# Two constant masks of an attention stage held in float32 in place of float16

## The reference

```
k_n = k / (norm(k) + 1e-6)
y[t] = q[t] @ state
v_old = k_n[t] @ state
state = state + beta[t] * outer(k_n[t], v[t] - v_old)
```

## Time and profile before

| | us |
|---|---|
| median of 3 runs | 1160.63 (1160.08 to 1163.29) |
| the profiled execution | 1159.56 |
| its span, first to last instruction | 1157.8 |
| TensorE matmul busy | 1044.8 (90%) |
| VectorE busy | 640.2 (55%) |
| ScalarE busy | 496.4 (43%) |
| GpSimd busy | 403.1 (35%) |
| mean granted TensorE clock | 0.931 |

### The profile page before, as it was taken

One profiled execution on the slowest core, in us unless ns is written; L12 is line 12 of the kernel. 1 busy time (PEld: TensorE's weight loads), 2 busy tenths in 40 slices (PEclk: granted clock), 3 DMA queues, 4 the chain that ended last, 5 costly groups with the idle time before them and its releaser, 6 DMA issues. The chain is left out here.

```text
span 1157.8 us, 28648 instructions
## 1 busy us (share of the span) xinstructions
PE 1044.8 (90%) x10998; PEld 898.0 (78%) x10998; DVE 640.2 (55%) x1051; ACT 496.4 (43%) x1007; POOL 403.1 (35%) x333
## 2 busy tenths in 40 slices
PE   3899898998989985999999999999994699999997
PEld 2788787888878874788787878878782588988886
DVE  5676576776777753645344343534435555445555
ACT  3564455655555643444233333423331434333433
POOL 5656446456546431005023050501302523212223
PEclk9798789988889987999999999999997799999999
DMA  9223333223330004401010010100000813444423
GB/s 149 61 52 65 69 75 63 45 58 71 68 76 16 16 16 134 154 1 55 0 55 0 0 54 0 54 0 27 0 0 27 273 64 123 140 163 163 149 93 112
DMA packets 135378, 79.38 MB, mean 69 GB/s; under 512 B 78414, under 2 KB 126038, under 8 KB 135286
## 3 DMA queue, kind: packets, MB, share of 16 engines
q1 hardware_dynamic: 132886, 73.27, 23.4%
q10 hardware_dynamic: 2400, 4.72, 1.1%
HBM read 63.03 MB, written 14.94 MB: 67 GB/s over the span
## 5 line engine op out<-in xcount | busy, mean ns | idle before, releaser
L1170 DVE SCALAR_TENSOR_TENSOR m_act_r<-m_act_r,m_sb_col 128x512 f32<-128x512 f32 x96 | 84.0, 875 | 144.2 <-ACT m_act_r L1097 144.2
L1488 POOL TENSOR_TENSOR e_w_lo<-e_w_raw,e_w_hi 128x384 fp32r<-128x384 f32 x64 | 72.6, 1144 | 177.2 <-ACT e_w_hi L1510 177.2
L1097 ACT ACTIVATE m_act_r<-m_hid 128x512 f32<-128x512 f32 x96 | 57.0, 594 | 142.1 <-PE m_hid L1215 140.2
L1173 DVE SCALAR_TENSOR_TENSOR m_g_lo<-m_act_r,m_sb_col,m_g_hi 128x512 fp32r<-128x512 f32 x96 | 75.5, 786 | 76.0 <-ACT m_g_hi L1100 76.0
L1215 PE MATMUL m_hid<-m_x_hi,m_w_hi 128*128 128x512 f32 x288 | 113.1, 393 | 4.3 <-DVE m_x_lo L1158 4.3
L1100 ACT ACTIVATE m_g_hi<-m_act_r,m_sb_col 128x512 fp32r<-128x512 f32 x96 | 69.5, 724 | 102.6 <-DVE m_act_r L1170 102.6
L1215 PE MATMUL m_out<-m_g_hi,m_w_hi 128*128 128x512 f32 x288 | 112.9, 392 | 0.5 <-DVE m_g_lo L1173 0.3
L1045 POOL TENSOR_TENSOR m_sq<-m_x_f 128x512 f32<-128x512 f32 x15 | 15.2, 1041 | 282.0 <-ACT m_x_f L1107 282.0
L1215 PE MATMUL m_hid<-m_x_lo,m_w_hi 128*128 128x512 f32 x288 | 112.9, 392 | 0.0
L1215 PE MATMUL m_hid<-m_x_hi,m_w_lo 128*128 128x512 f32 x288 | 112.8, 392 | 0.0
L1215 PE MATMUL m_out<-m_g_hi,m_w_lo 128*128 128x512 f32 x288 | 112.2, 390 | 0.0
(11 more groups left out here) (225 smaller groups left out, 2674.4 us busy)
## 6 DMA issues: line engine op xcount, KB each, us to landing
e_w_raw<-in_moe_w_dram SPq DMA_DIRECT2D x64, 384.0 KB, 7.1
a_b_rows<-in_beta_dram SPq DMA_DIRECT2D x48, 128.0 KB, 3.6
e_x_raw<-x2T_scratch SPq DMA_DIRECT2D x8, 768.0 KB, 4.7
out_dram<-e_acc SPq DMA_DIRECT2D x7, 768.0 KB, 3.5
a_k_raw<-in_k_dram SPq DMA_DIRECT2D x24, 192.0 KB, 3.8
a_q_raw<-in_q_dram SPq DMA_DIRECT2D x48, 96.0 KB, 3.0
a_v_raw<-in_v_dram SPq DMA_DIRECT2D x24, 192.0 KB, 3.6
xT_scratch<-a_y_T SPq DMA_DIRECT2D x48, 96.0 KB, 2.0
```

What stands on the lines that cost most here:

```text
L1097: nc.scalar.activation(act_r[:, f % RING, :], hid[f % RING][:, :], ACT.Relu).then_inc(s["relu_ready"], 1)
L1170: nc.vector.scalar_tensor_tensor(out=r, in0=r, scalar=sb_col[:, 0:1], in1=r, op0=ALU.mult, op1=ALU.mult).then_inc(s["sq_ready"], 1)
L1173: nc.vector.scalar_tensor_tensor(out=g_lo[:, f % RING, :], in0=r, scalar=sb_col[:, 1:2], in1=f32(g_hi[:, f % RING, :]), op0=ALU.add, op1=A ...
L1488: nc.gpsimd.tensor_tensor(w1_lo[:, :, c], w1_raw[:, :, c], f32(w1_hi[:, :, c]), ALU.subtract).then_inc(s["w1_lo_ready"], 1)
```

## The change

Two masks are held in float32. `minus_small` replaces `minus_small_h` and is made in float32; `off_blocks` reads `upper_off`, which is there in float32 already, in place of its float16 copy. The copy `upper_off_h` is still made. The outputs stay float16, and the values of the masks are 0, 1 and -1 in both types.

```diff
-        minus_small_h = sb("a_minus_small_h", [C, C], F16)
+        minus_small = sb("a_minus_small", [C, C], F32)
...
-            nc.vector.tensor_scalar(minus_small_h[:, :], small_blk[:, :], -1.0, None, ALU.mult).then_inc(s["made_v"], 1)
+            nc.vector.tensor_scalar(minus_small[:, :], small_blk[:, :], -1.0, None, ALU.mult).then_inc(s["made_v"], 1)
...
-                    nc.vector.tensor_tensor(l_small[:, gs(g), :], l_hi[:, gs(g), :], blk(minus_small_h), ALU.mult
+                    nc.vector.tensor_tensor(l_small[:, gs(g), :], l_hi[:, gs(g), :], blk(minus_small), ALU.mult
                                             ).then_inc(sg["l_small"][i], 1)
...
-                    nc.vector.tensor_tensor(l_offT[:, gs(g), :], l_hi[:, gs(g), :], blk(upper_off_h), ALU.mult
+                    nc.vector.tensor_tensor(l_offT[:, gs(g), :], l_hi[:, gs(g), :], blk(upper_off), ALU.mult
                                             ).then_inc(sg["l_offT"][i], 1)
```

## The result

The changed kernel takes 1173.72 us (median of 4 runs, 1172.81 to 1174.53), the kernel before beside it 1161.86. The ratio is 1.0095, with a 95% interval from 1.0074 to 1.0116: 11 us, or about 1%, slower. The forecast was 14.6 us or 1.3% slower, 1175.2. The two profiled executions lie 14.6 us apart (1159.56 and 1174.12), but that this is the forecast's own number is chance: the profiled execution of the kernel before lies 2.3 us under its median, that of the changed kernel 0.4 above.

A forecast was written before the change was run, and what follows sets the result against it. TensorE was taken to set the pace in the attention stage, standing still 62 of 442 us, partly for VectorE. Terms 8.4 + 4.2 + 2.0 = 14.6 us gave 1174.2 profiled, 1175.2 as median; range 1160 to 1192.

The forecast's parts named there:

- The bare price: Each of 48 VectorE mask products takes 0.54 us more, 1.22 alone, 1.09 behind GpSimd; 26 us of VectorE time.
- rival 4: The mixed float16 and float32 product is no slower, or all is hidden: 1160.6 us; chance 0.12.
- The first race: Second `l_small` against GpSimd's `l_lo` in A phases: VectorE wins, `l_small` ends almost 1 us earlier, `l_lo` takes 3.17.
- A phases: Seven of the attention stage's eleven phases, those not at the rolled loop's edge: 7 x 1.2 = 8.4 us.
- the prologue: From 25.38 us on, both `off_blocks` end later (30.1 for 28.6, 32.5 for 30.5): 2.0 us.
- B phases: Four phases at the rolled loop's edge: GpSimd keeps the lead, residual 1.06 late, 4 x 1.06 = 4.2 us.
- The second race: Second `off_blocks` against the other `l_lo` in A phases: GpSimd wins by 0.16 us, third `small_out` 1.2 us late.
- rival 1: VectorE wins the second race too, an A phase costs only 0.25: 1168.6 us; chance 0.20.
- TensorE's waits: Attention stage: wait for `l_small` gone, for `residual` above 2 us, a new one for `small_out` near 1 us.
- The clock: TensorE's granted clock in the attention stage, mean 0.87, left as it is in the sum.
- rival 2: More half clock in the attention stage: 10 us on top if half-clock time grows by a third, 1185 us; chance 0.18.
- rival 3: Faster: `l_small` wait and clock fall go in A phases, 1149.7 us with all seven; chance 0.08.

The follow-up runs named there:

- repeated run: The changed kernel, unaltered, run again beside its variants: 1172.39 us, 1.0099 of the kernel before.
- second pair: Kernel before and changed kernel, GpSimd's `vb` first, `l_lo` of group 1 waiting for `off_blocks` of group 1: 1126.94 us (float16), 1135.24 us (float32).
- first pair: Kernel before and changed kernel, GpSimd's `vb` first, `l_lo` of group 1 waiting for `off_blocks` of group 0: 1128.62 us (float16), 1137.70 us (float32).

## Why the prediction was right

**The bare price** was taken at 1.22 us alone and 1.09 behind GpSimd, from the experts' float32 rows. Measured 1.216 and 1.09. One float32 input is enough to lose the float16 pace; rival 4 falls. The Trainium skill's Vector Engine (DVE) Microarchitecture Reference, section 5.1, asks for two bytes in every source and the destination before a product of two tensors runs at two elements a cycle, and the trace agrees (1.216 us for the mix, 0.683 for float16 alone).

**The first race** was to go to VectorE in A phases, by a tie seen once in the prologue. It did in all seven, with `l_small` at 1.23, `l_lo` at 3.08 to 3.17 (forecast 3.17) and `vb` at 2.45 (forecast 2.46). The B phases went as written, `l_small` waiting and `off_blocks` ending 1.08 behind `vb`.

**The second race** was to go to GpSimd by 0.16 us in all seven. It went to GpSimd in five; in the two others VectorE was 0.01 us ahead, as at 170.79 against 170.80:

```profile
170.79 1.21 DVE L534 TENSOR_TENSOR a_t_small_x<-a_l_hi,a_upper_off 128x1024 f16<-128x1024 f16 x1
170.80 3.20 POOL L281 TENSOR_TENSOR a_l_lo<-a_l_full,a_l_hi 128x1024 f16<-128x1024 f32 x1
```

So forecast and rival 1 were both partly true, and this is the term that was mis-sized: 7 x 1.2 = 8.4 us. From one first `l_small` of a phase to that of the next (the last phase up to the stage's last copy), the seven A intervals of the two traces differ by 6.6 us in all, 8.5 in the five in which VectorE lost the race and -2.0 in the two in which it won. The sum is near because two errors cancel: a phase with a lost race cost 1.7 us and not 1.2, and one with a won race gave 1.0 back where 0.25 was to be paid. That part is luck. The B intervals differ by 4.8 (forecast 4.2), single ones by anything from -0.2 to 2.4, and the prologue's by 1.6 (forecast 2.0): 13.0 in place of 14.6, before the 2 us of the start. The medians show 11.9, and the kernel before, at 1161.86 beside the changed one, was 1.2 us above the 1160.63 that the forecast started from, so 1173.72 lies closer to 1175.2 than the 11.9 does to 14.6.

**TensorE's waits** came as named: the wait for `l_small` gone in A phases, 2.51 us for the residual ("above 2"), 0.80 for `small_out` ("near 1"). A small one of 0.3 us for ScalarE's copy, late with the masks, was named as a way to be wrong; it came, 2.1 us in all, and in A phases lies in front of the longer wait for the residual.

**The clock** was left out of the sum. Its mean over the stage stayed at 0.87 (0.86 in the repeated run): neither rival 2 nor rival 3. TensorE's busy time grew by 1.6 us, by 3.7 in the repeated run, so leaving the clock out cost little. The experiments show that it was the uncertain part: kernels that took the stalls away had 0.94 to 0.95 there, and by the traces most of what a lost second race costs is half-speed clock, which the 1.2 us of the sum did not hold.

**What fell short** was a picture behind the sum: I had expected the price to be made mostly by waits for the port. The second pair, whose products run without such waits, keeps 6.6 to 8.3 of the 11 to 12 us, so that by estimate more than half is VectorE's queue itself.

The best version measured is the kernel before with GpSimd's order of the second pair, 0.9725 of its time, faster than both kernels and level with the first pair's 0.9728.

## What to carry to other kernels

Where two engines share a port, a row's duration is its work plus its wait: look for rows of one form with several durations, and line their ends up with the other engine's. Then follow who is first at each meeting, because a change of half a microsecond can turn a wait round; give the engine that is not the bottleneck the wait, and the order of its work, held by semaphores, can be worth more (2.7% here) than the width of an operand (1%). Holding a constant operand in the wider type was not free here, although nothing else was converted.

## What the runs showed that was not expected

- An instruction of VectorE released by a semaphore at the end of GpSimd's loses the next turn for the port too (30 us in this kernel), while one already waiting for the port gets it next.
- The race is decided by hundredths of a microsecond: VectorE, started 0.01 us ahead, ran in 1.21; started 0.03 behind (420.70 against 420.67), in 3.17.
- A VectorE `tensor_scalar` of 128x128 with one SBUF input, float32 to float32, took 1.48 us when GpSimd's product had started before it and ended 0.08 behind that product; otherwise it took 0.34 or 0.56. So a one-input instruction can wait for GpSimd as well, and a product of VectorE for GpSimd's one-input `affine_select` (1.62 in place of 1.22).
- Removing 2 us of stalls per phase gave 3: the half-speed time of the stage shrank with them (mean clock 0.87 to 0.94 and 0.95).
